# A fused attention, soft mixture of experts and squared-ReLU feed-forward kernel: ACT takes its relus before the high parts of the step ahead, the last group goes product by product only in its last step, and the beginning gets more matmuls on the identity

## The reference, cut to what matters

```
scores = scale * q @ k.T                        # 4 batches, 8 heads, 576 tokens, head width 64
attn   = softmax(where(0 <= i - j < 128, scores - slope * |i - j|, -1e9)) @ v
x      = attn, as 2304 rows of 512
logits = x @ phi                                # 32 slots, 4 for each of 8 experts
slot_input = softmax over tokens(logits).T @ x
slot_out   = relu(slot_input @ w1[e]) @ w2[e]   # 512 -> 1024 -> 512 for each expert
y      = softmax over slots(logits) @ slot_out
h      = relu(y @ w_in)                         # 512 -> 2048
out    = (h * h) @ w_out                        # 2048 -> 512
```

## Time and profile before

| what | value |
|---|---|
| median of 3 runs | 422.62 us (421.81 to 422.99) |
| the profiled execution's own time | 421.05 us |
| its span, first to last instruction | 419.3 us |
| PE busy | 397.3 us (95%) |
| DVE, ACT, POOL busy | 284.7, 266.8, 98.1 us |
| DMA | 61.39 MB, mean 146 GB/s |

### The profile page before, as it was taken

How to read it: one execution, slowest core, us unless ns; L and a number is a source line. 1 busy time by engine, 2 the same in 40 slices (tenths; PEclk the granted TensorE clock), 3 DMA queues, 4 the chain that set the end, 5 groups by cost and what they waited for, 6 DMA issues and landing times.

```text
span 419.3 us, 8850 instructions
## 1 busy us (share of the span) xinstructions
PE 397.3 (95%) x3305; PEld 324.1 (77%) x3305; DVE 284.7 (68%) x738; ACT 266.8 (64%) x610; POOL 98.1 (23%) x94
## 2 busy tenths in 40 slices
PE   6799999999989999979899999999999999999977
PEld 5588888787767654423578888889999999899976
DVE  4788888888854544112899994766786868686752
ACT  3889898989853321001967878776767666677720
POOL 4677787878550010000052000000000000000000
PEclk9899999999999999989999999999999999999999
DMA  6678999987724799999700101001010101010011
GB/s 185 160 235 280 250 324 256 300 252 249 191 98 148 270 368 390 405 382 386 262 2 1 52 0 52 0 12 40 2 51 2 52 0 50 0 42 8 2 50 52
DMA packets 49877, 61.39 MB, mean 146 GB/s; under 512 B 25520, under 2 KB 33712, under 8 KB 48304
## 3 DMA queue, kind: packets, MB, share of 16 engines
q1 hardware_dynamic: 49296, 60.37, 42.8%
q10 hardware_dynamic: 544, 0.52, 0.4%
HBM read 56.16 MB, written 4.72 MB: 145 GB/s over the span
## 4 chain that ended last, share of the span: by engine, by line
PE 53%; ACT 18%; DVE 17%; issue 6%; DMA 5%; ACTq 0%; DVEq 0%
PE psum L1257 6%; PE psum L1301 6%; PE psum L1283 5%; ACT step_raw L1146 5%; ACT step_raw L1142 4%; PE psum L1544 4%; ACT step_hi L1126 4%; PE psum L1545 4%; PE psum L1546 4%; DMA ring<-in_moe_w 4%; DVE step_raw L897 4%; PE psum L1451 3%; ACT probs L994 3%; DVE step_raw L894 2%; PE psum L1216 2%
## 5 line engine op out<-in xcount | busy, mean ns | idle before, releaser
L1126 ACT CAST step_hi<-step_raw 128x896 fp32r<-128x896 f32 x48 | 42.8, 940 | 41.4 <-DVE step_raw L900 41.4
L994 ACT ACTIVATE probs<-probs,row_min 128x256 f32<-128x256 f32 (+1 forms) x128 | 60.0, 471 | 13.5 <-DVE row_min L639 13.5
L581 POOL TENSOR_TENSOR probs<-probs,row_inv 128x1024 f32<-128x1024 f32 x31 | 59.2, 1930 | 23.9 <-DVE row_inv L690 23.9
L887 DVE TENSOR_TENSOR step_lo<-step_raw,step_hi 128x896 fp32r<-128x896 f32 x48 | 50.2, 1088 | 17.7 <-ACT step_hi L1126 17.5
L1572 PE MATMUL psum<-t_hi,step_lo 128*128 128x256 f32 x192 | 54.0, 281 | 0.0
L1571 PE MATMUL psum<-t_lo,step_hi 128*128 128x256 f32 x192 | 53.9, 281 | 0.0
L1570 PE MATMUL psum<-t_hi,step_hi 128*128 128x256 f32 x192 | 53.9, 281 | 0.0
L639 DVE CUSTOM_DVE_ANT_0 probs<-psum,rel 128x256 f32<-128x256 f32 (+1 forms) x128 | 42.1, 385 | 4.0 <-PE psum L1257 4.0
L1570 PE MATMUL psum<-wout_hi,step_hi 128*128 128x256 f32 x144 | 40.6, 282 | 3.1 <-DVE step_lo L887 2.6
L1572 PE MATMUL psum<-wout_hi,step_lo 128*128 128x256 f32 x144 | 40.5, 281 | 0.0
L1571 PE MATMUL psum<-wout_lo,step_hi 128*128 128x256 f32 x144 | 40.4, 281 | 0.0
(11 more groups left out here) (180 smaller groups left out, 861.2 us busy)
## 6 DMA issues: line engine op xcount, KB each, us to landing
ring<-in_moe_w SPq DMA_DIRECT2D x16, 1024.0 KB, 6.0
ring<-in_moe_w SPq DMA_DIRECT2D x4, 2048.0 KB, 13.5
q_raw<-in_q SPq DMA_DIRECT2D x16, 256.0 KB, 3.2
v_in<-in_v SPq DMA_DIRECT2D x32, 128.0 KB, 2.6
ring_late<-in_moe_w SPq DMA_DIRECT2D x2, 2048.0 KB, 9.3
ring_x<-in_moe_w SPq DMA_DIRECT2D x2, 2048.0 KB, 8.0
win_sb<-in_moe_w_in SPq DMA_DIRECT2D x4, 1024.0 KB, 13.9
wout_raw<-in_moe_w_out SPq DMA_DIRECT2D x4, 1024.0 KB, 14.3
```

Source lines behind the costliest of these rows:

```text
L581: nc.gpsimd.tensor_tensor(probs[:, par, h, 0:4, :], probs[:, par, h, 0:4, :], row_inv[:, par, 4 * h:4 * h + 4].unsqueeze(2).to_broadcast([ ...
L994: nc.scalar.activation(t, t, ACT.Exp, bias=row_min[:, par, one:one + 1], scale=-1.0, accum_out=row_sum[:, par, one:one + 1]).then_inc(exp_ ...
L1126: nc.scalar.copy(step_hi[j][:, i, :, :], step_raw[j][:, i, 1:8, :]).then_inc(hi_done, 1)
```

## The change

Four edits, in the order of the program.

1. Six matmuls on the identity instead of three at the start, and six transposes of the identity behind the first pair's transposes, before the first scores.
2. DVE's `take_tails(2)` moves ahead of `invert(0, 0)`, which waits for the first pair's exponentials.
3. On ACT, in `next_steps`, `high_steps` of the step before stands behind the two relus, ahead of the square.
4. In group 8 step 2 goes like steps 0 and 1, and only step 3 goes product by product; product 3 still does all eight chunks at the end.

```diff
@@ DVE, attention step @@
+                if n == 0:
+                    take_tails(2)
                 if 0 <= n < NP:
                     invert(n, 0)
-                if 0 <= n < NP - 2:
+                if 1 <= n < NP - 2:
                     take_tails(n + 2)
@@ DVE, take_out @@
                 if is_last(n):
-                    dve.wait_ge(l2_used, NB * n + L2_AT + NB - 2)
+                    dve.wait_ge(l2_used, NB * n + L2_AT + NB - 1)
@@ ACT, next_steps @@
-                if j > 0:
-                    high_steps(n, j - 1)
-                elif not isinstance(n, int) or n > CONV:
-                    high_steps(n - 1, NB - 1)
...
                     nc.scalar.activation(step_raw[j][:, i, 0:4, :],
                                          psum[:, i, :].rearrange("p (s x) -> p s x", x=P), ACT.Relu).then_inc(relu_done, 1)
+                if j > 0:
+                    high_steps(n, j - 1)
+                elif not isinstance(n, int) or n > CONV:
+                    high_steps(n - 1, NB - 1)
                 act.wait_ge(relu_done, FU * n + 2 * j + 2)
@@ PE, beginning @@
                     transpose_tails(0)
+                    for _ in range(6):
+                        nc.tensor.transpose(psum[:, 0, 0:P], ident[:, :], ident[:, :])
...
             pe.wait_ge(consts_ready, 3)
-            for _ in range(3):
+            for _ in range(6):
                 mm(psum[:, 0, 0:P], ident[:, :], ident[:, :], start=True, stop=True)
@@ PE, last group @@
-                    for c in range(0 if x == 3 else KH // 2, KH):
+                    for c in range(0 if x == 3 else KH - 2, KH):
                         last = product(n, par, x, c)
...
-                    if is_last(n) and j == NB // 2:
+                    if is_last(n) and j == NB - 1:
                         last_products(n, par)
                         return
```

## The result

The changed kernel takes 407.37 us in the median of four executions (406.85 to 411.49), the kernel before 422.63 us (421.81 to 422.99, four executions). The ratio is 0.9658, 95% interval 0.9605 to 0.9710: faster by 3.4%, 14 to 15 us. The profiled execution took 406.96 us with a span of 405.2 us, against 421.05 and 419.3 before. Beside the experiments the kernel before was measured again, 57 executions in three sets with medians of 421.00, 421.42 and 421.94 us; by these the gain is 13.6 to 14.6 us.

What follows compares the result with a forecast made beforehand. PE nearly bound it, delayed by a closed ring over ACT and DVE. Terms 4.7 + 3.3 + 1.0 = 9.0 us gave 412.0 from the profiled 421.05, 413.6 from the median 422.62; forecast 413.0, range 410.5 to 416.5.

Steps and rivals of the forecast that it cites:

- The ring: Groups 3 to 7: casts, relus, square, sums form a closed 5.54 us turn; relus first make it 4.44, gaining 4.7 us.
- One sign named beforehand: Changed profile: 21.9 to 22.0 us from one group's hidden step to the same of the next.
- So a step that waits for nothing takes 0.50 + 42 x 0.1178 = 5.45 us: Odd steps on PE: 0.50 us to the first product, then 42 matmuls at 0.1178 us, taken as undisturbed.
- their term: Groups 3 to 7: five groups of 21.96 us each, where they took 114.41 us together.
- Rival (b): From 277.5 us on: PE, always supplied, runs 1092 matmuls at 0.109 instead of 0.119, 10 us more, 403; 2 in 100.
- The entry: Start of group 3: product 4 waits for DVE's later copy of group 2's result, stall 0.3 us, between 0 and 0.7.
- The last group: Group 8: waits of 2.6 and 0.4 us go, hidden start to last matmul start 20.4 instead of 23.7, gaining 3.3 us.
- The beginning: Start of the kernel: added work brings the clock's rise forward; 1.0 us gained, from -0.6 to 2.1.
- The term "1.1 us": First scores: first part of added work slow, 0.5 us late, then scores quick; 1.1 us gained.
- that low stretch at 18 us: First pair's transposes from 20.0 us: 0.55 us quicker if less idling keeps the clock up, as much lost if slowed later.
- upper end, 2.1: Start of the kernel: the largest gain allowed for, 2.1 us, in a span from -0.6.
- Edit 2 was put at -0.1 us: Second pair's scores go some 2 us sooner, but PE's next first-pair work waits for POOL; -0.1 us taken.

Runs made afterwards that it cites:

- relu_only: Kernel before with only the relus moved ahead of the casts on ACT; 412.43 us, ratio 0.9787.
- last_only: Kernel before with only the last group changed; 418.47 us, ratio 0.9932.
- warm_only: Kernel before with only the added matmuls and transposes of the beginning; 419.60 us, ratio 0.9962.
- wait_s3_done: Changed kernel with each hidden step on PE also waiting for DVE's first sum of the step before; 416.41 us, ratio 0.9876.
- even_128: Changed kernel with step 2's two buffers 128 bytes higher and nothing else; 409.58 us, ratio 0.9718.
- ring_shift192: Changed kernel with all SBUF tiles but the odd steps' buffers 192 bytes higher; 411.54 us, ratio 0.9792.
- late_shift192: Changed kernel with the odd steps' buffers, and the ring part sharing their room, 192 bytes lower; 411.84 us, ratio 0.9797.
- even_shift: Changed kernel with step 2's buffers 192 bytes higher and the high part of step 0 64 bytes higher; 405.85 us, ratio 0.9624.
- even_64: Changed kernel with step 2's buffers 64 bytes higher and step 0's high part 192 bytes higher; 406.78 us, ratio 0.9676.

## Why the forecast was right in its places and too small in its size

**The ring (edit 3): right.** In groups 3 to 7 PE felt ACT and DVE through the relus alone. Ahead of the casts they wait for PE by 1.1 to 1.8 us, all hidden rows have 0.64 us, and no low part is late. relu_only shows that this edit does it by itself. One sign named beforehand did not come: a group takes 21.52 us (295.88 to 317.40) and not 21.9 to 22.0.

**"So a step that waits for nothing takes 0.50 + 42 x 0.1178 = 5.45 us": this step failed.** The stretch from 329.31 to 334.14 in the earlier trace rows was read as a step without a wait, and its spacing as PE's own. Within the step PE did not wait, but its hidden matmuls ahead had: ACT's relus out of their banks ran from 327.83 to 328.91, and the hidden step had begun at 328.81. Their row is 0.66 us long and not the 0.64 of a step that finds its banks empty, and so in every other odd step of groups 3 to 7, 0.65 to 0.67 us. In the even steps without a bracket the hidden matmuls take 0.59 us to the first product (289.23 to 289.82), though no wait is in their rows either. Unhindered, an odd step takes 0.48 + 42 x 0.1134 = 5.24 us, and a group 0.48 x 4 + 84 x 0.1134 + 84 x 0.1200 = 21.5 us instead of 21.96. Five times 0.4 to 0.5 is the 2.2 us that the five groups gave beyond their term. The trace of before had a counter-example that I did not look for. In group 8 no hidden step stands ahead of step 1's products, and there the spacing is the quick one from the first matmul on (timeline of PE, before):

```profile
397.90 0.28 PE L1570 MATMUL psum<-t_hi,step_hi 128*128 128x256 f32 x1
...
401.86 0.28 PE L1572 MATMUL psum<-t_hi,step_lo 128*128 128x256 f32 x1
```

35 spacings of 0.1131 us. Rival (b) had this mechanism, PE's pace not being its own, and priced it at 0.109 for every matmul, 10 us. It was given 2 in 100 with the words "the spacings above come from stretches without a wait", which is the very step that failed. It happened for half of the matmuls and to 0.1134. The Trainium skill's page "TensorE: Matmul & The Clock Gate", section "Back-to-back issue gap", gives N / 2.4 + 2.5 ns for an isolated gap, by which an estimate for 256 columns is 109 ns; no step of any run here reached it, the quickest being 113.

**The entry: right.** In the first step of group 3 after its hidden step the mean spacing is 0.1298 instead of 0.120, 41 x 0.0098 = 0.4 us of stall, where 0.3 were taken.

**The last group (edit 4): right, 3.7 for 3.3 us.** Both waits went. The 0.4 us more is again the spacing: 0.113 in place of 0.118 us in step 1, and 0.115 in place of 0.119 in the 60 matmuls of the last part. relu_only and last_only show what the forecast did not say, that the wait of 2.6 us would have halved by edit 3 alone.

**The beginning: right in kind, 1.9 for 1.0 us.** The term "1.1 us" assumed that half of the added work is slow and the scores 0.5 us late. They were 0.08 us late: the added work filled the gap from about 3.9 to 4.8 that was there anyway, and its six transposes took 0.94 us in a gap of 0.66 us. The clock was up in time, so nearly all of the 1.55 us came, and 0.4 us more in the first pair's transposes, which no longer run at the low level. The forecast saw that low stretch at 18 us but tied it to edit 2. The traces tie it to neither edit: in warm_only PE stands idle 1.75 us ahead of the second pair's scores, nearly the 1.99 us of before, and the clock stayed up behind it; last_only, without either edit, kept it up, and wait_s3_done, with both, did not. So the 0.4 us are the luck of one execution. Why the clock fell in some and not in others is not shown. The forecast's upper end, 2.1, held. The Trainium skill's page "TensorE: Matmul & The Clock Gate", Part 1, has the low level as the default that sustained activity releases; the trace agrees, with 1.79 instead of 3.34 us. Edit 2 was put at -0.1 us; the third block shows 0.2.

**The clock in the experts: not foreseen.** The profiled execution of before contained a low-clock stretch of 1.6 us that that of the changed kernel didn't. The forecast counted from that execution as if it stood for the kernel; its executions at clock 1.0 take 419.4 us and not 421.05.

**Sum.** From the 9.0 us of the forecast to the 14.1 us of the profiled pair: 2.2 us the spacing and the hidden matmuls in groups 3 to 7 (less 0.1 for the stall), 0.4 us the last group, 0.9 us the start, 1.6 us the clock. The forecast also set 413.0 us, 1.0 above its sum, for the median, and the median lay 0.4 us above the profiled execution. The spacing is the largest term, but it alone would have left the forecast at 410.8 us; the clock and the start are the rest. The range took in 0.7 us of stall and 2.1 us for the start, and nothing for the spacing, since it was taken as measured. At equal clock the gain is 12.5 us.

**What stays open.** Why the odd steps of the kernel before go at 0.1178. Shown is that edit 3 alone brings 0.1134, that 0.1178 comes in most steps behind a stop of PE, though not in all, and that the places of the buffers matter. Read three by three, a product's matmuls (high by high, low by high, high by low) take 0.340 or 0.360 us in all but two cases of the changed kernel; in the kernel before they take mostly 0.353, 0.354 or 0.360, and about one in five another value near these. What sets these few values no run here shows. The part of ACT and DVE in it, whose work on the same buffers moved in the same experiments, was not tried apart.

## What to carry to other kernels

Before a spacing of matmuls is taken as PE's own, compare it between all stretches of the same shape, those right behind a short wait and those far from one; where they differ, the slower one may go with the wait. When an in-order engine has work that another waits for and work that nobody waits for, its order is worth more than its load: here the same instructions in another order took 9 of 419 us. In a kernel bound by 256-column matmuls try the buffers' places within 256 bytes against each other, which cost nothing and brought 2 us here and could have cost 3.4, and compare kernels at the same mean clock, since a single stretch of low clock is as large as such a gain.

## What the runs showed of the hardware that was not expected

The start-to-start time of the products' matmuls (256 columns, 128 x 128 loaded, granted clock 1.00), as the mean of a step of groups 3 to 7 (without the very first, with its stall), took few values: 0.1134, 0.1178 and 0.1200 us, each within 0.0004, and 0.1185 in step 2 of even_128. With the step's buffers and the weights `wout` and `t` beginning at the same place in their 256 bytes it was 0.1200 in all 38 steps of ring_shift192 and late_shift192 in groups 3 to 7 (without the first of group 3). A difference of 192 bytes gave 0.1134 in step 2 of even_shift, and one of 64 or 128 changed the pace of untouched steps too.

The clock fell behind one wait of 3.0 us and did not behind another of the same length at the same place. In ten of the 14 profiled executions, one for each kernel, it fell in the experts, at 179 to 182 us; those of the changed kernel, ring_shift192, late_shift192 and even_64 are the four where it did not. Over the executions of the kernel before the mean clock lay between 0.984 and 1.00. The time went with it at the ends and not between: the median was 419.4 us at 1.0, 421.4 at 0.995 and 0.996, 421.2 at 0.991 and 0.992, and 423.3 at 0.987 and 0.988. So only executions at the same mean clock should be set beside each other, and the mean clock does not give the time.
